# TensorE's loop over expert tiles, in rounds of four with an inner loop

## The reference

```python
# 1: retention, per head: scores * decay matrix, times v       (4 x 8 heads, 576 x 64)
scores = q @ k.T / sqrt(D);  ret = (scores * gamma ** (i - j) for i >= j) @ v
# 2: feed-forward                                              (2304 x 512, d_ff 1536)
x = (x @ w_a * (x @ w_b)) @ w_out
# 3: eight experts, one per token
logits = x @ w_gate + modality_bias[modality_id]
e_idx = argmax(logits, axis=1);  gate = softmax(logits)[e_idx]
for e in range(8):
    mask = e_idx == e
    out[mask] = gate[mask] * (relu(x[mask] @ w1[e]) @ w2[e])   # w1 512 x 1024, w2 1024 x 512
```

## Time and profile before

| | us |
|---|---|
| median of 3 runs (lowest, highest) | 808.96 (808.89, 810.09) |
| the profiled execution | 808.59 |
| its span, from the first to the last instruction | 806.8 |
| PE busy | 788.0 (98%) |
| DVE busy | 432.9 (54%) |
| ACT busy | 232.5 (29%) |
| POOL busy | 85.3 (11%) |

### The profile page before, as it was taken

The page is one execution under the profiler, slowest core; times in us unless marked ns, Lnnn a source line. Parts: engine busy times, 40 slices in busy tenths (PEclk is TensorE's granted clock), DMA queues, the critical chain, the costliest instruction groups (busy, mean ns, idle before and its releaser), DMA issues.

```text
span 806.8 us, 15685 instructions
## 1 busy us (share of the span) xinstructions
PE 788.0 (98%) x4983; PEld 702.0 (87%) x4984; DVE 432.9 (54%) x893; ACT 232.5 (29%) x429; POOL 85.3 (11%) x132
## 2 busy tenths in 40 slices
PE   7999999999999999999999999999999999999994
PEld 4888899999999999999999999998788888888882
DVE  3566543323334688886568888865744333352221
ACT  2433322323323232222343223242123212321110
POOL 3643000000000000000000000001121121212101
PEclk9999999999999999999999999999999999999998
DMA  9996241221212212124531221242453311111100
GB/s 216 235 241 118 73 139 39 79 67 50 78 43 76 76 43 78 45 72 124 177 92 40 78 70 47 75 161 93 153 188 109 138 39 39 52 39 39 40 13 14
DMA packets 101781, 72.34 MB, mean 90 GB/s; under 512 B 46190, under 2 KB 87278, under 8 KB 101616
## 3 DMA queue, kind: packets, MB, share of 16 engines
q1 hardware_dynamic: 82256, 51.44, 23.4%
q0 software_dynamic: 4384, 16.33, 5.8%
q10 hardware_dynamic: 15104, 4.07, 2.8%
HBM read 62.61 MB, written 9.74 MB: 90 GB/s over the span
## 4 chain that ended last, share of the span: by engine, by line
PE 94%; DVE 2%; DMA 2%; issue 1%; SPq 0%; POOL 0%; POOLq 0%; DVEq 0%
PE wide L1305 37%; PE bank L1788 23%; PE bank L1324 19%; PE bank L648 2%; PE bank L1812 2%; PE wide L713 2%; PE wide L680 2%; PE bank L703 1%; PE bank L620 1%; PE wide L261 1%; DMA qk_tail<-in_k_dram 1%; DMA xg<-x_rows,take 1%; PE bank L625 1%; PE wide L1336 1%; PE bank L340 1%
## 5 line engine op out<-in xcount | busy, mean ns | idle before, releaser
L1305 PE MATMUL wide<-x,wh 128*128 128x384 f32 x1136 | 289.3, 335 | 0.0
L1305 PEld LDWEIGHTS wide<-x,wh 128*128 128x128 f32 x1136 | 206.9, 188 | 6.1
L1305 PE MATMUL wide<-x,wl 128*128 128x384 f32 x568 | 190.7, 336 | 0.0
L1305 PEld LDWEIGHTS wide<-x,wl 128*128 128x128 f32 x568 | 106.6, 188 | 0.0
L1788 PE MATMUL bank<-expert_whl,hTh 128*128 (+1 forms) x304 | 96.2, 398 | 0.0
L1788 PE MATMUL bank<-expert_whl,xTh 128*128 (+1 forms) x296 | 93.1, 395 | 0.0
L1036 DVE TENSOR_TENSOR hid<-wide,a_sb 128x384 f32<-128x384 f32 x71 | 39.8, 560 | 98.9 <-PE wide L1305 58.2
L910 ACT ACTIVATE hh<-hid 128x384 fp32r<-128x384 f32 x72 | 37.8, 525 | 180.0 <-DVE hid L1036 169.9
L1324 PE MATMUL bank<-wh,hl 128*128 128x512 f32 x216 | 85.4, 396 | 0.0
L1324 PE MATMUL bank<-wl,hh 128*128 128x512 f32 x216 | 85.3, 395 | 0.0
L1324 PE MATMUL bank<-wh,hh 128*128 128x512 f32 x216 | 84.5, 391 | 0.0
(11 more groups left out here) (242 smaller groups left out, 919.7 us busy)
## 6 DMA issues: line engine op xcount, KB each, us to landing
expert_raw<-in_moe_w_dram SPq DMA_DIRECT2D x12, 1024.0 KB, 5.2
raw<-in_moe_w_a_dram SPq DMA_DIRECT2D x36, 256.0 KB, 3.2
raw<-in_moe_w_b_dram SPq DMA_DIRECT2D x36, 256.0 KB, 3.8
raw<-in_moe_w_out_dram SPq DMA_DIRECT2D x36, 256.0 KB, 2.7
q_nat<-in_q_dram SPq DMA_DIRECT2D x16, 256.0 KB, 5.3
k_nat<-in_k_dram SPq DMA_DIRECT2D x28, 128.0 KB, 4.8
x_rows<-x POOLq DMA_DIRECT2D x2, 1548.0 KB, 7.3
v_nat<-in_v_dram ACTq DMA_DIRECT2D x22, 128.0 KB, 5.0
```

What stands on the lines that cost most here:

```text
L1305: last = pe.matmul(ps[:, 0:HALF], w[par][m][:, P * t:P * t + P], x[:, g, part, t, cols], start=(k0 == 0), stop=(k0 == 3 * KD - 1))
```

## The change

PE's single loop over t from 3 to 27 becomes two nested ones. The outer makes ceil(25 / 4) = 7 rounds; a round whose first tile is not below the total is passed over as a whole. The inner makes four turns, each with the If on its own tile number. The tile's code is the same, as a function. The outer loop can reach tile numbers up to 30, so ST goes from SLOTS + 1 to SLOTS + 3 = 31, and three operations of make_plan that cover all but the last column are written with ST - 1 instead of SLOTS. The other engines' loops are as they were.

```diff
+ROUND = 4
...
-ST = SLOTS + 1
+ST = SLOTS + 3
...
-             dve.tensor_tensor(nxt[:, 0:SLOTS], tord[:, 1:ST], tord[:, 0:SLOTS], ALU.subtract),
+             dve.tensor_tensor(nxt[:, 0:ST - 1], tord[:, 1:ST], tord[:, 0:ST - 1], ALU.subtract),
...
-        with pe.Fori(OPEN, SLOTS) as t:
-            with pe.If(t < total):
-                loads = of_plan(pe, t, 0, 0, E - 1)
-                pe.wait_ge(s_xl, t + 1)
-                up_half(t, loads, 0)
-                before = of_plan(pe, t - 1, 0, 0, E - 1)
-                up_half(t, loads, 1)
-                with pe.If(t + 1 < total):
-                    ex.rows_transposed(pe, t + 1, ident)
-                down(t - 1, before)
-                hidden_transposed(t)
+
+        def tile(t):
+            loads = of_plan(pe, t, 0, 0, E - 1)
+            pe.wait_ge(s_xl, t + 1)
+            up_half(t, loads, 0)
+            before = of_plan(pe, t - 1, 0, 0, E - 1)
+            up_half(t, loads, 1)
+            with pe.If(t + 1 < total):
+                ex.rows_transposed(pe, t + 1, ident)
+            down(t - 1, before)
+            hidden_transposed(t)
+
+
+        with pe.Fori(0, -(-(SLOTS - OPEN) // ROUND)) as turn:
+            first = turn * ROUND + OPEN
+            with pe.If(first < total):
+                with pe.Fori(0, ROUND) as i:
+                    with pe.If(first + i < total):
+                        tile(first + i)
```

More of the change, by code:

```diff
@@ L1602, in make_plan @@
              dve.tensor_copy(plan[:, :, 0], q1[0:1, :]),
-             dve.tensor_scalar(nxt[:, 0:SLOTS], nxt[:, 0:SLOTS], float(QUARTERS), None, ALU.mult))
+             dve.tensor_scalar(nxt[:, 0:ST - 1], nxt[:, 0:ST - 1], float(QUARTERS), None, ALU.mult))
         link(dve.tensor_scalar(q1[:, :], q0[:, :], 1.0, float(QUARTERS), ALU.add, ALU.min))
         link(dve.tensor_scalar(q0[:, :], q0[:, :], float(QUARTERS), None, ALU.min),
-             dve.tensor_tensor(q1[:, 0:SLOTS], q1[:, 0:SLOTS], nxt[:, 0:SLOTS], ALU.max))
+             dve.tensor_tensor(q1[:, 0:ST - 1], q1[:, 0:ST - 1], nxt[:, 0:ST - 1], ALU.max))
         link(dve.tensor_scalar(nxt[:, :], tord[:, :], r["used"][:, 0:1], None, ALU.is_lt))
```

## The result

| | before | changed |
|---|---|---|
| median of six runs, us | 808.92 (808.5 to 810.09) | 804.67 (802.95 to 806.1) |
| profiled execution, us | 808.59 | 804.62 |
| its span, us | 806.8 | 802.8 |

The ratio is 0.9941 (95% interval 0.9929 to 0.9952): 4.8 us less, of 808.96 that is 804.2 (804.19). Put more simply, the two medians are 4.25 us apart and the means of the six runs 4.50. Measured again beside other kernels, the same file gave 0.9955 (0.9941 to 0.9969). Over all runs of this study the means are 808.97 (59 runs of the kernel before) and 804.95 (12 of the changed one), 4.02 us apart.

What follows compares the result with a forecast made beforehand. TensorE bounds the kernel almost throughout, with a 3.55 us gap at the loop's end. Terms -4.0 (end), +0.05 (entry) and +0.13 (tables) give -3.8 us: 804.8 profiled, 805.1 from the median; range for 8 in 10 804.2 to 806.5.

Steps and rivals of the forecast that it cites:

- The gap and its cause: Loop's end on PE: nine empty turns of 0.74 us leave 3.55 us idle; the change takes this to 0, at most 0.2.
- The sum for PE: Last tile's end on PE: filling 1.6 us, last products 5.5; PE ends at about 793.7, 5.1 us earlier.
- The way out of the loop: PE's sequencer after tile 18: 0.6 + 2.6 = 3.2 us (2.9 to 3.5) instead of 6.8, out at 786.3.
- What is late next: Last y: DVE's walk over its own empty turns sets it at 794.92; the end gains 4.0 of PE's 5.1 us.
- the entry: Start of tile 3 on PE, lead 0.6 us: 0.45 to 0.6 of added issue, taken as 0.05 us (0 to 0.2).
- The tables: ST from 29 to 31, one-hot operations ahead of `hot` and slot products: 0.13 us slower (0.05 to 0.25).
- Addition at every turn: Each tile's start on PE: `first + i` adds 0.1 us of issue, covered by the lead, so taken as 0.
- The lead of 1.2 us: Ordinary tile starts: PE's sequencer issues 1.2 us ahead of the first product, which covers the added loop instructions.
- what a round's start adds: Every fourth tile start on PE: leaving one round and entering the next adds 0.65 to 0.85 us, covered by the lead.
- With no idle stretch the clock has no reason in these rows to fall: PE behind the last transpose: filling at full clock takes 1.6 us instead of 2.22, last 24 products 5.5.
- 0.4 for how the runs spread: Allowance for run spread in the forecast's own range, 804.6 to 805.9 us.
- the rival in which DVE does not bind: Last y follows PE's end directly: gain 4.9 us, time 804.1; chance 0.06.

Runs made afterwards that it cites:

- rounds of two: The changed kernel with PE's inner loop making two turns a round (ROUND = 2) instead of four; ratio to before 0.9939, last transpose to y 8.77 us.
- rounds of one: The changed kernel with PE's inner loop making one turn a round (ROUND = 1); ratio to before 0.9996, last transpose to y 11.43 us.
- PE without filling: The changed kernel without the seven filling matmuls ahead of the last products (ENDING = 0); ratio to before 0.9946, last transpose to y 8.77 us.
- the added reads: The changed kernel with unused reads of the last tile's number at each tile start on PE's sequencer; ratio to before 1.0139 with three, 0.9939 with one.
- both engines in rounds: The changed kernel with DVE's loop, like PE's, in rounds of four; ratio to before 0.9932, median 803.79 us, last transpose to y 7.42 us.

## Why the prediction was right, and where its range was not

**The gap and its cause.** As forecast: nine empty turns at 0.74 us on the sequencer, of which the queue covered 3.3 us. The rounds of two and of one move the gap with the number of empty rounds: 0 (four), 0.92 (two), 3.84 us (one).

**The sum for PE.** The way out of the loop was put at 3.2 us; the sequencer was out at 785.9, 2.8 us behind 783.1, because an empty round costs 0.75 and not 0.9. PE's end was put at 793.7, it was 793.45.

**What is late next.** The forecast had y at 794.92; it began at 794.96. Three experiments hold it up: PE 1.1 us later changes nothing (rounds of two), PE without filling neither, and DVE in rounds moves y by 1.35 us. The profile has 804.62 where 804.8 was forecast, and the gain over all runs is 4.0 where 3.8 stood. In the two profiles the terms come out as -3.99 from the last transpose on (forecast -4.0), 0.00 at the entry and over the 16 tiles (0.05), and +0.12 from the feed-forward stage to the end of tile 2 (0.13); the stage itself began 0.11 earlier, which is not the change's.

**The tables and the tile starts.** 0.13 us for the tables, on the path as forecast. Addition at every turn: nothing, since it is fused with the copy of the loop register. The lead of 1.2 us stands, by the added reads, and what a round's start adds is 0.6 of it (0.65 to 0.85 had been put down), so half of it is left. At the entry only 0.2 us is left.

**The clock.** "With no idle stretch the clock has no reason in these rows to fall" held. But that 3.55 us of idling bring it down is not a fixed price: in three further profiles with a gap of that size (3.55, 3.55 and 4.11) it fell, in one with 3.84 it did not. When it falls it costs about 1.6 us: rounds of one without the fall took 11.43 with a gap longer by 0.29, so the kernel before would have taken 11.14 and took 12.76. By this estimate 1.6 of the 4.0 us gained are the clock, and a run of the kernel before in which it does not fall would be only 2.4 us slower than the changed one (11.14 - 8.77); how often that happens no run here tells. By the Trainium skill, TensorE: Matmul & The Clock Gate, Part 1, the chip watches activity in windows that run freely, so that the place of a transition shifts from run to run. The different outcomes for gaps of about one length agree with that.

**The range.** Here the prediction failed: the measured 804.2 (0.9941 of 808.96 is 804.19) lies under its low bound, if only by a hundredth. The term that was mis-sized is the spread: "0.4 for how the runs spread", from three runs of which the widest lay 1.2 apart. The runs of one kernel spread over 3 to 4 us, the 95% interval of one measurement is 0.9 to 1.1 us to either side, and two measurements of the same file lie 1.1 us apart: the first points to 804.2, the second to 805.3, all runs together to 804.9. Nor did the wider range help: it was to take in the rival in which DVE does not bind, whose own figure was 804.1, and ended at 804.2. What makes the spread is seen best at the start of the kernel, ahead of anything that the change touches. Windows of it in the kernel before and in the kernel with both engines in rounds:

```profile
12.00:15.50 3.50, 3.50 (x25) 2.08 (x24) 0.90 (x4) 0.24 (x1) 1.81 (x2) 0.52 1.32 238
15.50:18.50 3.00, 3.00 (x45) 2.46 (x44) 1.03 (x2) 1.25 (x3) 0.57 (x2) 0.99 1.25 236
```

```profile
12.00:15.50 3.50, 3.48 (x22) 1.93 (x23) 0.90 (x4) 0.28 (x1) 1.62 (x2) 0.50 1.32 233
15.50:18.50 3.00, 3.00 (x18) 2.58 (x18) 0.00 (x0) 1.36 (x3) 0.48 (x1) 0.53 1.25 221
```

At a clock of 0.99 PE got through 45 matmuls in 3 us, at 0.53 through 18. The half clock stood for 3.4 us in the one and for 6.8 in the other, and the feed-forward stage began at 98.1 and at 99.7. In the profile with three reads it did not stand at all there, and the stage began at 96.5. That is some 1.5 us for each such stretch, whichever kernel it is. It isn't all of the spread: the profile of rounds of one had the 3.4 us too and began the stage at 99.4, with 0.8 us of "issue" in the stage ahead that the others do not show. Among the runs of before and changed in the first measurement, two of six of the changed kernel had a mean clock of 0.996 (802.95 and 803.67); in the later measurements ten of the 53 runs of the kernel before had that clock, at 806.98 to 807.57, while its six runs in the first lay at 808.5 and above. How many runs of each kind fall into six is chance, and so, as far as these runs show, is most of the 0.8 us beyond 4.0. That the low clock at the start makes the spread is read from where the profiles part; no experiment took it away. A rival for the fast runs of the kernel before stands untested, that in them the clock did not fall behind the gap: the profile of rounds of one had a mean clock of 0.996 in just that way.

## What to carry to other kernels

A loop over a data-dependent count that runs to its static bound costs its empty turns on the sequencer of every engine, here 0.73 us each on PE and 0.53 on DVE; in this kernel they only showed where the queue ran dry, at the end. Look up when every other engine reaches the wait ahead of the next step: the second latest sets what a repair on the latest is worth (here 4.0 of 5.3 us), and the cure belongs on both. Before giving a range, look at how far single runs of the same kernel lie apart, and at the clock of each, and not only at its three runs' median.

## What the runs showed of the hardware that I had not expected

- A taken compare-and-branch holds PE's sequencer some 0.27 us to the next instruction (207 to 222 ns of its own, in the kernels before and changed), one that is not taken some 0.13 (65 to 86 ns).
- A multiply, an add and the copy of a loop register are one fused register operation of 37 to 50 ns: a round's `first` and a turn's `first + i` came at next to no cost beside the 29 ns copy that they replace.
- Issue time ahead of a tile's first product was free up to 1.2 us and cost in full beyond it: 2.0 us more cost 0.83 at an ordinary tile, 1.4 where a round had taken 0.6 of the lead, 1.80 at the entry.
- Idle stretches of 3.55 us (three profiles) and 4.11 us (one) on PE ended with the clock halved, one of 3.84 us did not; nor did one of 0.92 and one of 1.2 us.
- The releaser named for a wait can be the engine of the last semaphore (PE) where the waiting engine's own sequencer came later.
